# Split weights of two feed-forward layers kept in DRAM, in place of their sums alone

## The chip, the cores and the metric

The kernel runs on one core of one Trainium2 chip. The metric is the device time of one execution in microseconds; the median of several runs stands for a kernel. TensorE (PE) multiplies, VectorE (DVE), ScalarE (ACT) and GpSimd (POOL) work element by element, SyncE (SP) issues the DMA transfers between DRAM and SBUF, the memory on the chip.

## The reference

Attention with a memory term gives x, 2304 tokens by 512. Two feed-forward layers follow, all in float32:

```
g = x @ w_gate;  val = x @ w_val
x1 = (silu(g) * val) @ w_out          # 512 -> 1536 -> 512
h = x1 @ w_in                         # 512 -> 2048
g2 = h if h >= 1, 0 if h <= -1, else (h + 1)**2 / 4
out = g2 @ w_out2                     # 2048 -> 512
```

## The kernel before

The attention comes first, pair of heads by pair of heads. The feed-forward part is a hand-written schedule of 60 steps, in which each engine has its own program and waits for the others by semaphores.

**Tiling.** The tokens are cut into three superblocks of 768 for each layer: superblocks 0 to 2 are layer one (steps 0 to 35, 12 each), 3 to 5 are layer two (steps 36 to 59, 8 each). A step takes one block of weights of the up projection. It is multiplied by Strassen's scheme in Winograd's form: seven products of half size (`PRODUCTS`, L181) instead of eight. So the four quarters of a weight block need four sums besides (slots 4 to 7 of `wu_r`), and x needs four differences. The down projection works in groups of two tiles of weights (`wd_*`), 8 units of work a group, two groups behind the up projection (`LAG`).

**Three multiplications for one.** Float32 precision is reached by splitting each operand into a high part (rounded to fp32r) and a low part (the rest), and adding three matmuls: high by high, high by low, low by high (`three`, L1325). A matmul is 128x128 by 384 columns. A step has 42 matmuls for its products, and 24 (layer one, from step 4 on) or 48 (layer two) for units of the down projection. The last two groups follow after step 59.

**Splitting the weights.** The same weights serve three superblocks, and are loaded and split anew in each. For step u + 1, in step u: ScalarE writes the high parts of the up weights in three pieces (`up_high`, L718), GpSimd or VectorE subtract to get the low parts (`up_low`, L593 and L987; `pieces_of_pool`, L229, says which pieces are GpSimd's: one, but two or all three at a change of superblock). GpSimd and ScalarE do the same for the tiles of the down projection (`down_low` L604, `down_high` L727). `wu_l` and `wd_l` lie in the memory of `wu_r` and `wd_r`: the low part overwrites what was loaded.

**The sums.** `computed` (L204) tells in which steps GpSimd computes the four sums of the up weights (`up_sums_1`, `up_sums_2`): those of superblocks 0 and 3, and the first of superblocks 1 and 2. In the first of a layer SP stores them to DRAM (`keep_sums`, L470), and the splits that overwrite them wait for that store (L599, L992). In the others `load_up` (L461) loads the quarters and the kept sums.

**Buffers.** `wu_r`/`wu_l` has 3 buffers, `wu_h` 2, the tiles of the down projection 6 (3 groups). One SP program issues all loads and stores in the order of L510 to L523; a wait there holds up all that stands behind it.

**At a change of superblock** x of the next one is split too: seven high parts on ScalarE (`x_high`, L733), seven low parts on VectorE (`x_low`, L997), four differences on GpSimd (`x_sum`, L611, which waits at L618 for the last low part of the superblock before). VectorE also adds every unit of the down projection from PSUM into `xy` (`add_down`, L1111) and makes the low part of the hidden tiles (`hid_low`, L1095).

Of the kernel before, what the change touches and what calls it, by code (L numbers as in the profile page):

```python
# [1451 lines left out]
```

## Time and profile before

| | |
|---|---|
| median of 3 runs | 998.99 us (998.86 to 999.01) |
| profiled execution | 999.02 us |
| span of its trace | 997.2 us |
| TensorE, VectorE, ScalarE, GpSimd busy | 97%, 80%, 56%, 51% of the span |
| bytes moved by DMA | 116.13 MB, 116 GB/s over the span |
| granted TensorE clock | 1.000 of full speed |

The span runs from the first to the last instruction. Busy times of engines overlap. The records of matmuls overlap as well, since they are pipelined: the distance between the starts of two of them tells the pace, not their length.

### The profile page before, as it was taken

The numbers are of one execution on the slowest core, as the hardware profiler recorded it, in microseconds if no ns is written. First come the engines' busy times: TensorE is split into PE (matmuls) and PEld (weight loads), VectorE is DVE, ScalarE is ACT, GpSimd is POOL, SyncE is SP. The second block draws the span as 40 slices with busy tenths as digits, with TensorE's granted clock in tenths as the row PEclk, the third lists the DMA queues.
The fourth block names the chain that finished last, engine by engine and source line by source line (L and its number), as shares of the span: only waits on it lengthen the run. The fifth ranks groups of instructions, "written<-read, shape, count | busy, mean of one in ns | idle before, by whom it ended". The sixth has DMA issues, their size and how long they took to land.

```text
span 997.2 us, 19181 instructions
## 1 busy us (share of the span) xinstructions
PE 970.6 (97%) x6328; PEld 920.4 (92%) x6328; DVE 795.7 (80%) x1438; ACT 562.7 (56%) x1114; POOL 503.8 (51%) x407
## 2 busy tenths in 40 slices
PE   6999999999999999999999999999999999899998
PEld 4777777889999999999999999999989999899998
DVE  5888999567788677778667788888998888987776
ACT  5899998655446544454454454545654555545451
POOL 5677776176675233453234467576452526442331
PEclk9999999999999999999999999999999999999999
DMA  6545553333333332323333231323322431315211
GB/s 232 171 150 177 168 153 99 109 125 130 106 106 111 130 120 106 107 85 109 128 133 119 85 106 65 127 78 135 103 88 98 156 127 64 118 73 190 69 38 64
DMA packets 34782, 116.13 MB, mean 116 GB/s; under 512 B 4224, under 2 KB 4608, under 8 KB 34688
## 3 DMA queue, kind: packets, MB, share of 16 engines
q1 hardware_dynamic: 34544, 114.91, 34.2%
q8 instruction: 55, 0.90, 0.4%
q14 instruction: 39, 0.32, 0.1%
q10 hardware_dynamic: 144, 0.00, 0.0%
HBM read 100.14 MB, written 14.75 MB: 115 GB/s over the span
## 4 chain that ended last, share of the span: by engine, by line
PE 83%; DVE 6%; ACT 5%; issue 4%; DMA 1%; POOL 1%; SPq 0%; DVEq 0%; ACTq 0%; POOLq 0%
PE ps L1327 24%; PE ps L1329 23%; PE ps L1328 23%; PE ps L1302 5%; PE ps L1245 4%; ACT pt L716 3%; PE ps L1275 3%; DVE xt_l L1003 1%; DVE xy L1119 1%; DVE hid_l L1097 1%; DVE hid_r L1109 1%; ACT rown L695 1%; DMA qk<-qk_in 1%; DMA rbc<-rsums 0%; DVE negs L939 0%
## 5 line engine op out<-in xcount | busy, mean ns | idle before, releaser
L601 POOL TENSOR_TENSOR wu_l<-wu_r,wu_h 128x768 fp32r<-128x768 f32 (+1 forms) x75 | 142.0, 1901 | 396.3 <-ACT wu_h L725 396.3
L1327 PE MATMUL ps<-xt_h,wu_h 128*128 128x384 f32 x840 | 283.0, 337 | 5.9 <-DVE xt_l L1003 2.8
L1329 PE MATMUL ps<-xt_h,wu_l 128*128 128x384 f32 x840 | 280.8, 334 | 0.0
L1328 PE MATMUL ps<-xt_l,wu_h 128*128 128x384 f32 x840 | 280.7, 334 | 0.0
L1327 PE MATMUL ps<-hid_h,wd_h 128*128 128x384 f32 x672 | 226.2, 337 | 5.6 <-DVE xy L1119 5.3
L1329 PE MATMUL ps<-hid_h,wd_l 128*128 128x384 f32 x672 | 224.7, 334 | 0.0
L1328 PE MATMUL ps<-hid_l,wd_h 128*128 128x384 f32 x672 | 224.6, 334 | 0.0
L1119 DVE TENSOR_TENSOR xy<-xy,ps 128x384 f32<-128x384 f32 x288 | 157.2, 548 | 49.1 <-PE ps L1329 48.1
L803 ACT ACTIVATE hid_h<-hid_r 128x768 fp32r<-128x768 f32 x84 | 70.8, 843 | 199.1 <-DVE hid_r L1093 142.9
L1327 PEld LDWEIGHTS ps<-xt_h,wu_h 128*128 128x128 f32 x840 | 157.6, 188 | 13.7 <-issue 12.0
L1328 PEld LDWEIGHTS ps<-xt_l,wu_h 128*128 128x128 f32 x840 | 157.7, 188 | 0.0
L1329 PEld LDWEIGHTS ps<-xt_h,wu_l 128*128 128x128 f32 x840 | 157.7, 188 | 0.0
L607 POOL TENSOR_TENSOR wd_l<-wd_r,wd_h 128x512 fp32r<-128x512 f32 x84 | 136.6, 1639 | 15.1 <-ACT wd_h L730 13.9
L1327 PEld LDWEIGHTS ps<-hid_h,wd_h 128*128 128x128 f32 x672 | 126.1, 188 | 11.3 <-issue 6.9
L994 DVE TENSOR_TENSOR wu_l<-wu_r,wu_h 128x512 fp32r<-128x512 f32 x105 | 121.4, 1156 | 6.9 <-DMA kept<-wu_r 3.9
L1328 PEld LDWEIGHTS ps<-hid_l,wd_h 128*128 128x128 f32 x672 | 126.2, 188 | 0.0
L1329 PEld LDWEIGHTS ps<-hid_h,wd_l 128*128 128x128 f32 x672 | 126.1, 188 | 0.0
L725 ACT ACTIVATE wu_h<-wu_r 128x512 fp32r<-128x512 f32 (+1 forms) x180 | 118.9, 694 | 0.0
L1097 DVE TENSOR_TENSOR hid_l<-hid_r,hid_h 128x768 fp32r<-128x768 f32 x84 | 86.6, 1030 | 37.2 <-ACT hid_h L803 37.1
L695 ACT ACTIVATE rown<-negs,nmax 128x576 f32<-128x576 f32 (+3 forms) x128 | 77.1, 605 | 14.9 <-DVE nmax L939 14.9
L818 ACT ACTIVATE tmp<-hb,nhalf 128x768 f32<-128x768 f32 x48 | 45.1, 940 | 50.8 <-issue 45.9
L1103 DVE SCALAR_TENSOR_TENSOR tmp<-tmp 128x768 f32<-128x768 f32 x48 | 54.9, 1144 | 19.3 <-ACT tmp L818 18.7
(84 smaller groups left out, 1323.8 us busy)
## 6 DMA issues: line engine op xcount, KB each, us to landing
wu_r<-w_up SPq DMA_DIRECT2D x60, 512.0 KB, 4.6
wd_r<-w_down SPq DMA_DIRECT2D x42, 512.0 KB, 3.7
wu_r<-kept SPq DMA_DIRECT2D x38, 512.0 KB, 5.6
kept<-wu_r SPq DMA_DIRECT2D x19, 512.0 KB, 4.6
qk<-qk_in SPq DMA_DIRECT2D x15, 640.0 KB, 5.1
nat<-nat_in SPq DMA_DIRECT2D x16, 384.0 KB, 3.1
vm<-vm_in SPq DMA_DIRECT2D x16, 320.0 KB, 3.6
rbc<-rsums SPq DMA_DIRECT2D x32, 144.0 KB, 3.0
```

Of the source, the lines that this page charges most:

```text
L601: nc.gpsimd.tensor_tensor(wu_l[u % 3][:, a:b], wu_r[u % 3][:, a:b], wu_h[u % 2][:, a - 1:b - 1].bitcast(F32), ALU.subtract).then_inc(low_p ...
L607: nc.gpsimd.tensor_tensor(wd_l[:, t % 6], wd_r[:, t % 6], wd_h[:, t % 6].bitcast(F32), ALU.subtract).then_inc(wd_lo, 1)
L695: nc.scalar.activation(head_rows(j)[:, h + (i == 1), D:D + w], negs[:, t % NEGS, 0:w], ACT.Exp, bias=nmax[:, p % 2, k:k + 1], scale=-1.0, ...
L725: nc.scalar.activation(wu_h[u % 2][:, a - 1:b - 1], wu_r[u % 3][:, a:b], ACT.Copy).then_inc(wu_hi[n], 1)
L803: nc.scalar.activation(hid_h[:, t % 6], hid_r[:, t % 6], ACT.Copy).then_inc(hh_done, 1)
L994: nc.vector.tensor_tensor(wu_l[u % 3][:, a:b], wu_r[u % 3][:, a:b], wu_h[u % 2][:, a - 1:b - 1].bitcast(F32), ALU.subtract).then_inc(low_d ...
L1097: nc.vector.tensor_tensor(hid_l[:, t % 6], hid_r[:, t % 6], hid_h[:, t % 6].bitcast(F32), ALU.subtract).then_inc(hl_done, 1)
L1103: nc.vector.scalar_tensor_tensor(tmp[:, r], tmp[:, r], 1.0, tmp[:, r], ALU.min, ALU.mult).then_inc(s_done, 1)
L1119: nc.vector.tensor_tensor(y, y, o, ALU.add).then_inc(evac, 1)
L1327: nc.tensor.matmul(dst, w_hi, v_hi, start=start, stop=False, skip_group_check=onto)
L1328: nc.tensor.matmul(dst, w_hi, v_lo, start=False, stop=False, skip_group_check=onto)
L1329: return nc.tensor.matmul(dst, w_lo, v_hi, start=False, stop=stop, skip_group_check=onto)
```

## The change

In superblocks 0 and 3 the weights are loaded, summed and split as before. Then SP stores the high and low parts of all of them to four tensors in DRAM: seven slots for each up step (`keep_up`), two tiles for each group of the down projection (`keep_down`). In superblocks 1, 2, 4 and 5 the parts are read straight into the buffers from which TensorE takes them (`load_up_high`, the second branch of `load_up`, `load_down`), and no engine computes sums or splits for them; in these, TensorE waits for the loads at the first product of a step. The store of the sums (`keep_sums`) and its waits are gone. New waits: a load into a buffer waits until that buffer's store has landed; `up_high` and `down_high` wait until the store of the high part that they overwrite has landed. The first steps of superblocks 1 and 2 are no longer computed. The diff, cut to its core (the lines left out make the same conditions in the programs of ScalarE, VectorE and GpSimd, name semaphores and remove the old call of `keep_sums` in the attention):

```diff
@@ -104,7 +103,10 @@
 traw, o = place("traw", [P, 4, 2, HALF], F32, o)
-kept = nc.dram_tensor("kept", [S1 + S2, P, 4 * 2 * P], F32, kind="Internal").ap()
+kept_uh = nc.dram_tensor("kept_uh", [S1 + S2, P, 7 * 2 * P], F32, kind="Internal").ap()
+kept_ul = nc.dram_tensor("kept_ul", [S1 + S2, P, 7 * 2 * P], F32, kind="Internal").ap()
+kept_dh = nc.dram_tensor("kept_dh", [(NF1 + NF2) // 2, P, 2 * DM], F32, kind="Internal").ap()
+kept_dl = nc.dram_tensor("kept_dl", [(NF1 + NF2) // 2, P, 2 * DM], F32, kind="Internal").ap()
@@ -203,19 +209,15 @@
-    return superblock(u) in (0, NSB) or u < STEPS1 and u % S1 == 0
-def is_kept(u):
-    return superblock(u) in (0, NSB) and u > 0
+    return superblock(u) in (0, NSB)
+def computed_before(u):
+    return sum(computed(v) for v in range(u))
...
-    return 4 * sum(computed(v) for v in range(u))
-def kept_before(u):
-    return 16 * sum(is_kept(v) for v in range(u))
+    return 4 * computed_before(u)
@@ -223,7 +225,50 @@
-    return 16 * sum(1 if computed(v) else 2 for v in range(u % 3, u + 1, 3))
+    return 16 * (u // 3 + 1)
+def high_loads_until(u):
+    return 16 * sum(not computed(v) for v in range(u % 2, u + 1, 2))
+def kept_by(u):
+    return u % S1 if u < STEPS1 else STEPS1 + (u - STEPS1) % S2
+def stores_until(u, n):
+    return 16 * sum(computed(v) for v in range(u % n, u + 1, n))
+def down_computed(g):
+    return group_block(g) in (0, NSB)
+def down_computed_before(g):
+    return sum(down_computed(h) for h in range(g))
+def down_index(g):
+    return g % (NF1 // 2) if g < GROUPS1 else NF1 // 2 + (g - GROUPS1) % (NF2 // 2)
+def down_loads_until(g):
+    return 16 * sum(1 if down_computed(h) else 2 for h in range(g % 3, g + 1, 3))
+def down_kept_by(g):
+    return g % (NF1 // 2) if g < GROUPS1 else GROUPS1 + (g - GROUPS1) % (NF2 // 2)
+def down_stores_until(g):
+    return 16 * sum(down_computed(h) for h in range(g % 3, g + 1, 3))
+def tiles_split_until(t):
+    return 2 * down_computed_before(t // 2) + t % 2 + 1
@@ -458,28 +503,65 @@
     def load_up(u):
         at_least(sp, up, up_count(u - 3, 6))
+        if u >= 3 and computed(u - 3):
+            sp.wait_ge(up_kept_l[u % 3], stores_until(u - 3, 3))
         n = step_index(u)
-        sp.dma_start(wu_r[u % 3][:, 0:4], w_up[n].rearrange("p (k n) -> p k n", k=4)).then_inc(ld_up[u % 3], 16)
-        if not computed(u):
-            sp.wait_ge(sums_kept, kept_before(n + 1 if n < S1 else STEPS1 + n - S1 + 1))
-            sp.dma_start(wu_r[u % 3][:, 4:8], kept[n].rearrange("p (k n) -> p k n", k=4)).then_inc(ld_up[u % 3], 16)
-    def keep_sums(u):
-        sp.wait_ge(sums, sums_before(u) + 4)
-        sp.dma_start(kept[step_index(u)].rearrange("p (k n) -> p k n", k=4), wu_r[u % 3][:, 4:8]).then_inc(sums_kept, 16)
+        if computed(u):
+            sp.dma_start(wu_r[u % 3][:, 0:4], w_up[n].rearrange("p (k n) -> p k n", k=4)).then_inc(ld_up[u % 3], 16)
+        else:
+            sp.wait_ge(up_kept_l[kept_by(u) % 3], stores_until(kept_by(u), 3))
+            sp.dma_start(wu_l[u % 3][:, 1:8].bitcast(F32), kept_ul[n].rearrange("p (k n) -> p k n", k=7)).then_inc(ld_up[u % 3], 16)
+    def load_up_high(u):
+        at_least(sp, up, up_count(u - 2, 6))
+        if computed(u - 2):
+            sp.wait_ge(up_kept_h[u % 2], stores_until(u - 2, 2))
+        n = step_index(u)
+        sp.wait_ge(up_kept_h[kept_by(u) % 2], stores_until(kept_by(u), 2))
+        sp.dma_start(wu_h[u % 2][:].bitcast(F32), kept_uh[n].rearrange("p (k n) -> p k n", k=7)).then_inc(ld_uh[u % 2], 16)
+    def keep_up(u):
+        n = step_index(u)
+        for k in range(3):
+            sp.wait_ge(wu_hi[k], computed_before(u) + 1)
+        sp.dma_start(kept_uh[n].rearrange("p (k n) -> p k n", k=7), wu_h[u % 2][:].bitcast(F32)).then_inc(up_kept_h[u % 2], 16)
+        for k in range(3):
+            sp.wait_ge(*low_count(u, k))
+        sp.dma_start(kept_ul[n].rearrange("p (k n) -> p k n", k=7), wu_l[u % 3][:, 1:8].bitcast(F32)).then_inc(up_kept_l[u % 3], 16)
...
         at_least(sp, dn, UNITS * (g - 2))
-        n = g % (NF1 // 2) if g < GROUPS1 else NF1 // 2 + (g - GROUPS1) % (NF2 // 2)
-        s = 2 * (g % 3)
-        sp.dma_start(wd_r[:, s:s + 2], w_down[n].rearrange("p (k n) -> p k n", k=2)).then_inc(ld_dn[g % 3], 16)
+        if g >= 3 and down_computed(g - 3):
+            sp.wait_ge(dn_kept_l[g % 3], down_stores_until(g - 3))
+        n, s = down_index(g), 2 * (g % 3)
+        if down_computed(g):
+            sp.dma_start(wd_r[:, s:s + 2], w_down[n].rearrange("p (k n) -> p k n", k=2)).then_inc(ld_dn[g % 3], 16)
+            return
+        if down_computed(g - 3):
+            sp.wait_ge(dn_kept_h[g % 3], down_stores_until(g - 3))
+        by = down_kept_by(g)
+        sp.wait_ge(dn_kept_h[by % 3], down_stores_until(by))
+        sp.dma_start(wd_h[:, s:s + 2].bitcast(F32), kept_dh[n].rearrange("p (k n) -> p k n", k=2)).then_inc(ld_dn[g % 3], 16)
+        sp.wait_ge(dn_kept_l[by % 3], down_stores_until(by))
+        sp.dma_start(wd_l[:, s:s + 2].bitcast(F32), kept_dl[n].rearrange("p (k n) -> p k n", k=2)).then_inc(ld_dn[g % 3], 16)
+    def keep_down(g):
+        n, s = down_index(g), 2 * (g % 3)
+        sp.wait_ge(wd_hi, tiles_split_until(2 * g + 1))
+        sp.dma_start(kept_dh[n].rearrange("p (k n) -> p k n", k=2), wd_h[:, s:s + 2].bitcast(F32)).then_inc(dn_kept_h[g % 3], 16)
+        sp.wait_ge(wd_lo, tiles_split_until(2 * g + 1))
+        sp.dma_start(kept_dl[n].rearrange("p (k n) -> p k n", k=2), wd_l[:, s:s + 2].bitcast(F32)).then_inc(dn_kept_l[g % 3], 16)
@@ -512,10 +592,16 @@
             load_down(GROUPS1 + u - STEPS1)
-        if u > 0 and u + 1 < STEPS and is_kept(u + 1):
-            keep_sums(u + 1)
+        if u + 1 < STEPS and not computed(u + 1):
+            load_up_high(u + 1)
         if 0 < u and u + 2 < STEPS:
             load_up(u + 2)
+        if computed(u):
+            keep_up(u)
+        if u < STEPS1 and u % 2 == 1 and u >= 3 and down_computed((u - 3) // 2):
+            keep_down((u - 3) // 2)
+        if u >= STEPS1 + 2 and down_computed(GROUPS1 + u - STEPS1 - 2):
+            keep_down(GROUPS1 + u - STEPS1 - 2)
         if u > STEPS1 + S2 and (u - STEPS1) % S2 == LAG + 1:
@@ -593,17 +679,14 @@
         a, b = PIECES[n]
-        if computed(u):
-            pool.wait_ge(sums, sums_before(u) + (4, 3, 4)[n])
-        if n > 0 and is_kept(u):
-            pool.wait_ge(sums_kept, kept_before(u + 1))
-        pool.wait_ge(wu_hi[n], u + 1)
+        pool.wait_ge(sums, sums_before(u) + (4, 3, 4)[n])
+        pool.wait_ge(wu_hi[n], computed_before(u) + 1)
         nc.gpsimd.tensor_tensor(wu_l[u % 3][:, a:b], wu_r[u % 3][:, a:b], wu_h[u % 2][:, a - 1:b - 1].bitcast(F32),
...
-        pool.wait_ge(wd_hi, t + 1)
+        pool.wait_ge(wd_hi, tiles_split_until(t))
         nc.gpsimd.tensor_tensor(wd_l[:, t % 6], wd_r[:, t % 6], wd_h[:, t % 6].bitcast(F32),
@@ -719,14 +803,17 @@
         act.wait_ge(ld_up[u % 3], loads_until(u))
-        if computed(u):
-            at_least(act, sums, sums_before(u) + (0, 2, 4)[n])
+        at_least(act, sums, sums_before(u) + (0, 2, 4)[n])
         at_least(act, up, up_count(u - 2, 6))
+        if u >= 2 and computed(u - 2):
+            act.wait_ge(up_kept_h[u % 2], stores_until(u - 2, 2))
         nc.scalar.activation(wu_h[u % 2][:, a - 1:b - 1], wu_r[u % 3][:, a:b], ACT.Copy).then_inc(wu_hi[n], 1)
...
-        act.wait_ge(ld_dn[t // 2 % 3], 16 * (t // 6 + 1))
+        act.wait_ge(ld_dn[t // 2 % 3], down_loads_until(t // 2))
+        if t >= 6 and down_computed(t // 2 - 3):
+            act.wait_ge(dn_kept_h[t // 2 % 3], down_stores_until(t // 2 - 3))
         nc.scalar.activation(wd_h[:, t % 6], wd_r[:, t % 6], ACT.Copy).then_inc(wd_hi, 1)
@@ -879,7 +969,7 @@
             x_high(sb + 1, 0)
-        if more:
+        if split:
             if not fresh:
@@ -986,11 +1077,8 @@
         a, b = PIECES[n]
-        if computed(u):
-            dve.wait_ge(sums, sums_before(u) + 2 + n)
-        if is_kept(u):
-            dve.wait_ge(sums_kept, kept_before(u + 1))
-        dve.wait_ge(wu_hi[n], u + 1)
+        dve.wait_ge(sums, sums_before(u) + 2 + n)
+        dve.wait_ge(wu_hi[n], computed_before(u) + 1)
         nc.vector.tensor_tensor(wu_l[u % 3][:, a:b], wu_r[u % 3][:, a:b], wu_h[u % 2][:, a - 1:b - 1].bitcast(F32),
@@ -1334,8 +1423,12 @@
         sb = superblock(u)
-        pe.wait_ge(*low_count(u, piece_of(slot)))
-        pe.wait_ge(wu_hi[piece_of(slot)], u + 1)
+        if computed(u):
+            pe.wait_ge(*low_count(u, piece_of(slot)))
+            pe.wait_ge(wu_hi[piece_of(slot)], computed_before(u) + 1)
+        elif n == 0:
+            pe.wait_ge(ld_up[u % 3], loads_until(u))
+            pe.wait_ge(ld_uh[u % 2], high_loads_until(u))
         if u == first_of(sb):
@@ -1368,8 +1461,11 @@
         at_least(pe, hh_done, 2 * g + 2)
-        at_least(pe, wd_lo, 2 * g + 2)
-        at_least(pe, wd_hi, 2 * g + 2)
+        if down_computed(g):
+            pe.wait_ge(wd_lo, tiles_split_until(2 * g + 1))
+            pe.wait_ge(wd_hi, tiles_split_until(2 * g + 1))
+        else:
+            pe.wait_ge(ld_dn[g % 3], down_loads_until(g))
         at_least(pe, evac, n - 1)
...
```

## Rows read from the trace of the kernel before

**Rows 1.** Busy time of each engine, from the page.
```profile
PE 970.6 (97%) x6328; PEld 920.4 (92%) x6328; DVE 795.7 (80%) x1438; ACT 562.7 (56%) x1114; POOL 503.8 (51%) x407
```

**Rows 2.** Timeline of TensorE (start us, us long): first matmuls of steps, and the last.
```profile
184.86 0.44 PE L1327 MATMUL ps<-xt_h,wu_h 128*128 128x384 f32 x1
...
310.28 0.33 PE L1327 MATMUL ps<-xt_h,wu_h 128*128 128x384 f32 x1
...
322.52 0.33 PE L1327 MATMUL ps<-xt_h,wu_h 128*128 128x384 f32 x1
...
588.64 0.33 PE L1327 MATMUL ps<-xt_h,wu_h 128*128 128x384 f32 x1
...
718.54 0.33 PE L1327 MATMUL ps<-xt_h,wu_h 128*128 128x384 f32 x1
...
737.57 0.33 PE L1327 MATMUL ps<-xt_h,wu_h 128*128 128x384 f32 x1
...
867.50 0.33 PE L1327 MATMUL ps<-xt_h,wu_h 128*128 128x384 f32 x1
...
961.10 0.33 PE L1327 MATMUL ps<-xt_h,wu_h 128*128 128x384 f32 x1
...
976.85 0.41 PE L1327 MATMUL ps<-hid_h,wd_h 128*128 128x384 f32 x1
...
994.01 0.34 PE L1329 MATMUL ps<-hid_h,wd_l 128*128 128x384 f32 x1
```

**Rows 3.** Waits of TensorE (us in total, times, longest).
```profile
PE ps L1327 <- DVE xy L1119: 5.3, 10, 1.0
...
PE ps L1327 <- DVE xt_l L1003: 2.8, 5, 0.9
```

**Rows 4.** Timeline of VectorE in step 44.
```profile
721.12 0.95 DVE L1097 TENSOR_TENSOR hid_l<-hid_r,hid_h 128x768 fp32r<-128x768 f32 x1
...
722.86 0.54 DVE L1119 TENSOR_TENSOR xy<-xy,ps 128x384 f32<-128x384 f32 x1
...
723.32 2.14 DVE L1003 TENSOR_TENSOR xt_l<-traw,xt_h 128x768 fp32r<-128x768 f32 x1
...
725.39 2.03 DVE L1097 TENSOR_TENSOR hid_l<-hid_r,hid_h 128x768 fp32r<-128x768 f32 x1
```

**Rows 5.** Timeline of GpSimd in step 44.
```profile
722.34 6.22 POOL L601 TENSOR_TENSOR wu_l<-wu_r,wu_h 128x768 fp32r<-128x768 f32 x3 [4.62 <-ACT wu_h L725]
```

**Rows 6.** The costliest groups, from the page: splits of the weights.
```profile
L994 DVE TENSOR_TENSOR wu_l<-wu_r,wu_h 128x512 fp32r<-128x512 f32 x105 | 121.4, 1156 | 6.9 <-DMA kept<-wu_r 3.9
...
L601 POOL TENSOR_TENSOR wu_l<-wu_r,wu_h 128x768 fp32r<-128x768 f32 (+1 forms) x75 | 142.0, 1901 | 396.3 <-ACT wu_h L725 396.3
...
L607 POOL TENSOR_TENSOR wd_l<-wd_r,wd_h 128x512 fp32r<-128x512 f32 x84 | 136.6, 1639 | 15.1 <-ACT wd_h L730 13.9
...
L725 ACT ACTIVATE wu_h<-wu_r 128x512 fp32r<-128x512 f32 (+1 forms) x180 | 118.9, 694 | 0.0
```

**Rows 7.** Timeline of VectorE in step 2.
```profile
207.75 0.74 DVE L994 TENSOR_TENSOR wu_l<-wu_r,wu_h 128x512 fp32r<-128x512 f32 x1 [2.03 <-DMA kept<-wu_r]
```

**Rows 8.** Busy time by stretch; last columns: clock, DMA share, GB/s.
```profile
16.00:22.00 6.00, 4.92 (x38) 3.66 (x38) 5.13 (x17) 5.32 (x19) 5.08 (x7) 1.00 0.99 392
...
311.00:316.00 5.00, 4.91 (x28) 4.41 (x26) 4.80 (x7) 3.30 (x6) 0.00 (x0) 1.00 0.77 276
...
905.00:909.00 4.00, 4.00 (x25) 4.00 (x24) 3.16 (x5) 2.08 (x5) 3.80 (x3) 1.00 1.01 408
```

**Rows 9.** Timeline of SP in step 2.
```profile
204.77 0.33 SPq L473 DMA_DIRECT2D kept<-wu_r  x1
...
205.14 0.43 SPq L465 DMA_DIRECT2D wu_r<-w_up  x1
```

**Rows 10.** Timeline of GpSimd in step 47.
```profile
780.29 1.84 POOL L629 TENSOR_TENSOR traw<-xy 128x768 f32<-128x768 f32 x1
```

**Rows 11.** Timeline of VectorE in step 47.
```profile
780.95 2.00 DVE L1103 SCALAR_TENSOR_TENSOR tmp<-tmp 128x768 f32<-128x768 f32 x1
```

More of the change, by code:

```diff
@@ L235, in low_count @@
         def low_count(u, n):
-            pool = [n in pieces_of_pool(v - 1) for v in range(u + 1)]
-            return (low_pool if pool[u] else low_dve)[n], sum(p == pool[u] for p in pool)
+            pool = {v: n in pieces_of_pool(v - 1) for v in range(u + 1) if computed(v)}
+            return (low_pool if pool[u] else low_dve)[n], sum(x == pool[u] for x in pool.values())
         def raw_sum(sb, n):
@@ L665, in _ @@
                 for n in pieces_of_pool(u):
-                    if 0 < u and u + 1 < STEPS:
+                    if 0 < u and u + 1 < STEPS and computed(u + 1):
                         up_low(u + 1, n)
                 for t in down_tiles(u):
-                    down_low(t)
+                    if down_computed(t // 2):
+                        down_low(t)
                 if 0 < u and u + 2 < STEPS and computed(u + 2):
@@ L839, in _ @@
                     x_high(sb + 1, 0)
-                if u > 0:
+                if u > 0 and computed(u + 1):
                     up_high(u + 1, 1)
@@ L845, in _ @@
                 for t in down_tiles(u):
-                    down_high(t)
-                if u > 0:
+                    if down_computed(t // 2):
+                        down_high(t)
+                if u > 0 and computed(u + 1):
                     up_high(u + 1, 2)
@@ L862, in _ @@
                 more = u + 1 < STEPS
+                split = more and computed(u + 1)
                 ends = more and superblock(u + 1) != sb
@@ L881, in _ @@
                     x_high(sb + 1, 0)
-                if more:
+                if split:
                     if not fresh:
@@ L891, in _ @@
                 for t in down_tiles(u):
-                    down_high(t)
+                    if down_computed(t // 2):
+                        down_high(t)
                 if ends:
@@ L1142, in _ @@
                     x_low(sb, 5)
-                if u > 0 and 1 not in pieces_of_pool(u):
+                if u > 0 and computed(u + 1) and 1 not in pieces_of_pool(u):
                     up_low(u + 1, 1)
@@ L1147, in _ @@
                     add_down(n)
-                if u > 0 and 2 not in pieces_of_pool(u):
+                if u > 0 and computed(u + 1) and 2 not in pieces_of_pool(u):
                     up_low(u + 1, 2)
@@ L1166, in _ @@
                 more = u + 1 < STEPS
+                split = more and computed(u + 1)
                 ends = more and superblock(u + 1) != sb
@@ L1181, in _ @@
                     x_low(sb, 4)
-                if more and 1 not in pieces_of_pool(u):
+                if split and 1 not in pieces_of_pool(u):
                     up_low(u + 1, 1)
@@ L1192, in _ @@
                 add_down(units[3])
-                if more and 2 not in pieces_of_pool(u):
+                if split and 2 not in pieces_of_pool(u):
                     up_low(u + 1, 2)
```

12 lines of the change are left out of this document (7 added, 5 removed).

## The prediction

> **What bounds the kernel now.** First the busy shares: TensorE is at 97%, the next engine at 80% [rows 1]. A busy share is no proof for pipelined matmuls, so next the timeline of TensorE. Its 4536 feed-forward matmuls run from 184.86 to 994.01 us [rows 2]. Steps 53 to 58 show the pace when nothing is late: 961.10 - 867.50 = 93.60 us for 6 x 90 matmuls, 0.1733 us each [rows 2]. At that pace 4535 intervals are 786.1 us; the stretch is 809.15 us. So TensorE is held up for 23.1 us, and no change beside the matmuls can bring more. Nothing is said of the attention before, which the change leaves as it is, one early transfer apart.
>
> Where the 23.1 us lie, by superblock (length less matmuls x 0.1733, all starts from [rows 2]): superblock 0, where the weights of layer one are split for the first time, 125.42 - 696 x 0.1733 = 4.8. Superblocks 1 and 2 together, 278.36 - 1584 x 0.1733 = 3.8; of it step 12 alone 12.24 - 11.44 = 0.8. Superblock 3, 129.90 - 124.80 = 5.1. Superblocks 4 and 5, 258.31 - 249.60 = 8.7; of it step 44 alone 19.03 - 15.60 = 3.4, and step 52 repeats it. The tail, 17.16 - 16.47 = 0.7. The waits of TensorE in feed-forward name VectorE: 5.3 us for the adds into xy and 2.8 us for the low parts of x [rows 3]. So VectorE is what comes late.
>
> Why is it late in step 44, where it has no weight to split (there GpSimd takes all three pieces)? VectorE's subtract of 128x768 took 0.95 us at 721.12. The same at 725.39 took 2.03, and the low part of x at 723.32 took 2.14, while GpSimd ran three subtracts without a break from 722.34 on [rows 4, 5]. The adds that read PSUM stay at 0.54 beside it [rows 4]. So GpSimd's work on the weights stretches VectorE's operations on SBUF alone.
>
> **What goes away.** In the four superblocks that are no longer computed go two thirds of the splits. Group by group [rows 6]: VectorE keeps 37 of 105 `up_low`, 68 x 1.16 = 79 us gone; GpSimd keeps 23 of 75 and 28 of 84 `down_low`, 52 x 1.90 + 56 x 1.64 = 191 us gone; ScalarE keeps 60 of 180 `up_high`, 120 x 0.69 = 83 us gone, and 56 `down_high`. None of this is on TensorE, so only what it does to the 23.1 us counts.
>
> Superblocks 1 and 2: apart from the two change steps, 3.8 - 1.6 = 2.2 us go, less 0.2 in step 35, which still splits for step 36. Of the 0.8 in a change step most is the chain from the last product to the low part of x, which stays; I take 0.25 each as gained. Sum 2.5 of 3.8.
>
> Superblocks 4 and 5: without GpSimd, the two operations of step 44 lose 1.19 and 1.08 us, and the three low parts of x behind them their share; that is the size of the step's 3.4. The steps 47 to 50 lose two `up_low` each. I keep 1.1 us as left and count 7.6 of 8.7.
>
> Superblock 0: in steps 2 and 3 VectorE waited for the store of the sums before it could overwrite them (2.03 us in step 2 [rows 7]). That wait falls: the new stores follow the split. Bound 0 to 2 us for each of two steps; TensorE felt it through one add, and I take 0.65 each, 1.3. Superblock 3 and the tail keep theirs.
>
> **What is added, all of it on the SP queue.** A step's seven slots are 917,504 bytes a part. In superblock 0 each step stores 1.84 MB and loads 0.52, and every second step loads 0.52 and stores 1.05 for a group: 6.3 MB in two steps of 11.44 us. Later steps load 1.84 MB, and 1.05 every second step. What can the queue move? With a backlog the rows show 392 GB/s for loads (16 to 22 us) and 408 for the output's store (905 to 909); without one, 276 (311 to 316) [rows 8]. The new queue has a backlog, so I take 400 and keep 276 for the range. At 400 two steps need 15.7 of 22.9 us. TensorE kept its pace under 408 GB/s (25 matmuls in 4 us [rows 8]), so more traffic slows no matmul: nothing, with that cover.
>
> The new waits. `load_up(u + 2)` now waits until the low part of step u - 1 has landed in DRAM; behind it on SP stand `keep_up(u)`, `keep_down` and the next `load_down`. A store's fixed part: issued at 204.77, it let VectorE go at 207.75 [rows 7, 9], 2.98 us, less 0.52 MB at 408 = 1.3, leaves 1.7 us. From the first issue at about 188.6 us: (0.52 + 1.84) MB at 400 is 5.9, plus 1.7, so the load for step 3 goes out near 196.3, and 7.6 us later, at 203.9, the one for step 4, which before went out at 205.14 [rows 9]. So at 400 nothing is late; at 276 it would be 10.2 us a turn, the load for step 4 at 209, four us late, and GpSimd's sums, ScalarE's and VectorE's splits wait behind it. I take 0; range 0 to 7 us. ScalarE's `up_high` waits for the high store of two steps earlier, which is queued ahead of that low store and lands first.
>
> In the other superblocks TensorE waits at product 0 for both loads. The worst is an even step: 1.05 MB and the high part, 1.97 MB, issued at its start, are there after 5.0 + 1.7 us, at 276 after 8.8, of 11.44. Layer two has 15.6. Nothing.
>
> Sum: 2.5 + 7.6 + 1.3 = 11.4 us. The profiled execution took 999.02 us, 0.03 above the median of the runs, so the forecast is 999.02 - 11.4 = 987.6 for both. Differences of 0.2%, 2 us, are about what a measurement of this kernel tells from none.
>
> **Rivals.** *Slower: the SP queue becomes the bound in superblock 0.* Until the high part for step 13 is there it must move 12 x 1.84 + 5 x 1.05 (stores) + 15 x 0.52 + 1.05 + 4 x 0.92 (loads) = 39.8 MB, from 188.3 to about 320.8 (322.52 before [rows 2] less 1.7), in 132.5 us. Six times, at even steps, nothing is queued behind the waiting load: 6 x 1.7 = 10 us. At 400 that is 110 us, 22 to spare; at 276, 154, so TensorE waits 22 us in steps 1 to 13, and 999 + 22 - 11 = 1010. It decides below 39.8 / (132.5 + 11.4 - 10) = 297 GB/s. For it: 276 is a real row. Against: that window had a DMA share of 0.77, the queue was not full, and stores show 408 [rows 8]. Chance 0.09. *No difference:* rates near 300 give back what is gained, 997 to 1001; 0.05.
>
> *The four differences of x bunch up.* GpSimd's `x_sum` no longer stand behind splits; all four for the next superblock can run as soon as the last low part of x is done, late in step 44. One of 1.84 us at 780.29 stretched VectorE's operation at 780.95 to 2.00 [rows 10, 11]. Four of them are 7.4 us in a step where VectorE has least to spare, worth up to half of that, in both layers: 991. By the Trainium skill, page "SBUF — State Buffer", section "SBUF: two separate sides", the two engines share a port pair as an exclusive lock, held for a whole instruction, against VectorE operations with two SBUF inputs; the rows agree (2.03 against 0.95, PSUM adds at 0.54 [rows 4]), and by the page the bunch would stop each such operation in turn. Chance 0.08.
>
> *VectorE's own work is the limit* at steps 44 and 52, and the stretching only filled idle time. Then 2 x 3.4 us of the 7.6 stay, and the time is 994. Against it: the operations in [rows 4] follow each other without a gap. Chance 0.08.
>
> **Numbers.** The forecast has 0.70: 987.6, and from 985.4 (all of superblocks 4 and 5 and 2 us more in superblock 0 gained) to 990. With the two smaller gains the range is 985.4 to 994.5 and holds 0.86. Faster 0.86, same 0.05, slower 0.09.
>
> **What would show it.** Right: steps 44 and 52 within 0.8 us of 15.60, no stretched subtracts there, superblock 3 still some 5 us over, DMA shares near 1 in superblock 0 with SP's waits ending before TensorE's. Wrong: a wait of TensorE for a DMA at the start of steps 12 to 14, or steps 1 to 4 longer than now because the sums start late; a queue under 300 GB/s with a backlog; or step 44 unchanged with GpSimd idle.

## The result and the profile after

The changed kernel takes 990.39 us in the median of 4 runs (990.22 to 991.28), the kernel before on the same chip 998.92 (998.60 to 999.01). The ratio is 0.9917 with an interval from 0.9900 to 0.9934: faster by 8.5 us, where 11.4 were forecast. The profiled execution took 990.56 us, 988.7 of them in the span, at a granted clock of 1.000.

The page of the changed kernel, busy time of the engines and bytes moved (beside [rows 1]):

```profile
PE 965.2 (98%) x6328; PEld 921.2 (93%) x6328; DVE 709.6 (72%) x1370; ACT 463.1 (47%) x938; POOL 309.8 (31%) x291
...
DMA packets 46156, 204.72 MB, mean 207 GB/s; under 512 B 5488, under 2 KB 5872, under 8 KB 46064
```

The costliest groups of the changed kernel, splits of the weights (beside [rows 6]):

```profile
L684 POOL TENSOR_TENSOR wu_l<-wu_r,wu_h 128x768 fp32r<-128x768 f32 (+1 forms) x23 | 44.1, 1922 | 79.8 <-ACT wu_h L810 79.7
L690 POOL TENSOR_TENSOR wd_l<-wd_r,wd_h 128x512 fp32r<-128x512 f32 x28 | 43.6, 1568 | 42.6 <-ACT wd_h L817 42.3
...
L810 ACT ACTIVATE wu_h<-wu_r 128x512 fp32r<-128x512 f32 (+1 forms) x60 | 39.7, 692 | 0.6 <-PE ps L1418 0.6
L1082 DVE TENSOR_TENSOR wu_l<-wu_r,wu_h 128x512 fp32r<-128x512 f32 x37 | 37.3, 1009 | 1.4 <-ACT wu_h L810 1.4
```

The counts are those worked out from the code: 23, 28, 60 and 37. GpSimd lost 194 us of busy time, ScalarE 100, VectorE 86; the time fell by 8.5. Busy time off the critical path is not worth its length. What counts stands in the timeline of TensorE in the changed kernel (beside [rows 2]):

```profile
184.47 0.44 PE L1416 MATMUL ps<-xt_h,wu_h 128*128 128x384 f32 x1
...
309.80 0.33 PE L1416 MATMUL ps<-xt_h,wu_h 128*128 128x384 f32 x1
...
321.60 0.33 PE L1416 MATMUL ps<-xt_h,wu_h 128*128 128x384 f32 x1
...
585.07 0.33 PE L1416 MATMUL ps<-xt_h,wu_h 128*128 128x384 f32 x1
...
715.35 0.33 PE L1416 MATMUL ps<-xt_h,wu_h 128*128 128x384 f32 x1
...
731.97 0.33 PE L1416 MATMUL ps<-xt_h,wu_h 128*128 128x384 f32 x1
...
749.73 0.33 PE L1416 MATMUL ps<-xt_h,wu_h 128*128 128x384 f32 x1
...
843.33 0.33 PE L1416 MATMUL ps<-xt_h,wu_h 128*128 128x384 f32 x1
...
858.93 0.33 PE L1416 MATMUL ps<-xt_h,wu_h 128*128 128x384 f32 x1
...
968.13 0.33 PE L1416 MATMUL ps<-hid_h,wd_h 128*128 128x384 f32 x1
...
985.47 0.34 PE L1418 MATMUL ps<-hid_h,wd_l 128*128 128x384 f32 x1
```

Read as in the prediction, each stretch less its matmuls x 0.1733 us:

| stretch | lost before | lost after | gain | forecast |
|---|---|---|---|---|
| superblock 0 (184.47 to 309.80) | 4.8 | 4.7 | 0.1 | 1.3 |
| superblocks 1, 2 (to 585.07) | 3.8 | 0.7 | 3.1 | 2.5 |
| superblock 3 (to 715.35) | 5.1 | 5.5 | -0.4 | 0 |
| superblocks 4, 5 (to 968.13) | 8.7 | 3.2 | 5.5 | 7.6 |
| tail (to 985.47) | 0.7 | 0.9 | -0.2 | 0 |

So 8.2 us of the 23.1 came back and 14.9 stayed. Two terms were missed: superblock 0 gave 0.1 in place of 1.3, and superblocks 4 and 5 gave 2.1 less. Of the 3.2 that they still lose, step 44 has 731.97 - 715.35 - 15.60 = 1.0, and step 45, which lost nothing before, 749.73 - 731.97 - 15.60 = 2.2. Steps 47 to 50 and step 52 (843.33 to 858.93) are at 15.60.

**Step 45.** VectorE in steps 44 and 45 of the changed kernel (beside [rows 4]):

```profile
719.54 0.95 DVE L1091 TENSOR_TENSOR xt_l<-traw,xt_h 128x768 fp32r<-128x768 f32 x1
720.41 0.95 DVE L1185 TENSOR_TENSOR hid_l<-hid_r,hid_h 128x768 fp32r<-128x768 f32 x1
...
727.99 2.25 DVE L1191 SCALAR_TENSOR_TENSOR tmp<-tmp 128x768 f32<-128x768 f32 x1
730.16 0.54 DVE L1207 TENSOR_TENSOR xy<-xy,ps 128x384 f32<-128x384 f32 x1
730.63 2.12 DVE L1197 TENSOR_TENSOR hid_r<-hb,tmp 128x768 f32<-128x768 f32 x1
...
733.13 2.13 DVE L1191 SCALAR_TENSOR_TENSOR tmp<-tmp 128x768 f32<-128x768 f32 x1
...
735.65 2.12 DVE L1185 TENSOR_TENSOR hid_l<-hid_r,hid_h 128x768 fp32r<-128x768 f32 x1
```

and GpSimd in the same stretch (beside [rows 5]):

```profile
723.92 3.70 POOL L690 TENSOR_TENSOR wd_l<-wd_r,wd_h 128x512 fp32r<-128x512 f32 x2 [12.06 <-ACT wd_h L817]
727.58 1.84 POOL L712 TENSOR_TENSOR traw<-xy 128x768 f32<-128x768 f32 x1
729.57 2.37 POOL L712 TENSOR_TENSOR traw<-xy,traw 128x768 f32<-128x768 f32 x1
731.89 2.56 POOL L712 TENSOR_TENSOR traw<-xy 128x768 f32<-128x768 f32 x1
734.41 2.55 POOL L712 TENSOR_TENSOR traw<-xy,traw 128x768 f32<-128x768 f32 x1
```

The two operations that took 2.14 and 2.03 us now take 0.95, as forecast. Then the four `x_sum` run without a break from 727.58 to 736.96, after the last low part of x and right behind GpSimd's last two splits of down weights, and four VectorE operations take 2.12 to 2.25. They seem to take turns. The one begun at 730.63 lies in a difference that ends at 731.94; 0.95 more gives 732.89, and it ended at 732.75. The next difference begins at 731.89; 1.84 from 732.75 gives 734.59, and it ended at 734.45. The add that reads PSUM stays at 0.54. That is what the lock in the Trainium skill, page "SBUF — State Buffer", section "SBUF: two separate sides", would give.

**Superblock 0.** SP, the loads of the quarters for steps 3, 4 and 5 in the changed kernel, and one of down weights between them (beside [rows 9]):

```profile
196.72 0.33 SPq L514 DMA_DIRECT2D wu_r<-w_up  x1
...
198.05 1.50 SPq L548 DMA_DIRECT2D wd_r<-w_down  x1
...
206.67 0.33 SPq L514 DMA_DIRECT2D wu_r<-w_up  x1
...
215.32 0.33 SPq L514 DMA_DIRECT2D wu_r<-w_up  x1
```

GpSimd there, the first sum for step 4:

```profile
211.03 0.74 POOL L668 TENSOR_TENSOR wu_r<-wu_r 128x256 f32<-128x256 f32 x1 [1.71 <-DMA wu_r<-w_up]
```

Busy time by stretch (beside [rows 8]; the last columns are clock, DMA share and GB/s):

```profile
200.00:212.00 12.00, 11.53 (x65) 10.91 (x64) 7.55 (x11) 6.45 (x12) 8.57 (x9) 1.00 0.83 319
212.00:224.00 12.00, 10.38 (x59) 9.78 (x58) 9.45 (x12) 7.56 (x13) 10.04 (x10) 1.00 0.85 312
190.00:310.00 120.00, 117.08 (x668) 115.24 (x667) 87.48 (x122) 61.27 (x102) 73.90 (x61) 1.00 0.83 305
```

and the first waits of TensorE in step 3, from its timeline:

```profile
215.12 0.41 PE L1416 MATMUL ps<-xt_h,wu_h 128*128 128x384 f32 x1 [0.91 <-ACT u2s L875]
...
217.10 0.44 PE L1416 MATMUL ps<-xt_h,wu_h 128*128 128x384 f32 x1 [0.70 <-POOL wu_l L684]
```

The load for step 4 went out at 206.67, not at 203.9. GpSimd waited 1.71 us for it, its sums came late, ScalarE's high parts behind them, and TensorE lost 0.91 and 0.70 us in step 3, where the kernel before lost 0.19 and 0.24 at the same two places. In return the two waits of TensorE for `hb`, a block that VectorE adds up from the products, 0.43 us each in steps 3 and 4 before, are gone.

Waits of TensorE over the whole execution (beside [rows 3]):

```profile
PE ps L1416 <- DVE xy L1207: 4.9, 11, 1.1
...
PE ps L1416 <- DVE xt_l L1091: 0.4, 1, 0.4
```

The wait for the low parts of x fell from 2.8 to 0.4 us; that for `xy` is still there, but it is another one: what is left of it lies outside the steps 47 to 50 and 52, which are at pace now.

### The profile page after: what moved, and what is told of

It is laid out like the page before. It is cut to its first block, busy times and chain, and to the rows that moved or that the text cites. A ratio compares the mean times of both kernels' runs of the same rounds, so it can differ in the third digit from the quotient of the medians.

```text
span 988.7 us, 18774 instructions
## 1 busy us (share of the span) xinstructions
PE 965.2 (98%) x6328; PEld 921.2 (93%) x6328; DVE 709.6 (72%) x1370; ACT 463.1 (47%) x938; POOL 309.8 (31%) x291
## 2 busy tenths in 40 slices
DMA packets 46156, 204.72 MB, mean 207 GB/s; under 512 B 5488, under 2 KB 5872, under 8 KB 46064
## 4 chain that ended last, share of the span: by engine, by line
PE 84%; ACT 5%; issue 4%; DVE 4%; DMA 2%; POOL 1%; ACTq 0%; DVEq 0%; SPq 0%; POOLq 0%
PE ps L1416 24%; PE ps L1417 24%; PE ps L1418 24%; PE ps L1391 5%; PE ps L1334 4%; ACT pt L800 3%; PE ps L1364 3%; DMA kept_ul<-wu_l 1%; DVE xt_l L1091 1%; DVE xy L1207 1%; ACT rown L779 1%; DMA betas<-beta 1%; DVE hid_l L1185 1%; ACT tmp L905 0%; DMA wu_r<-w_up 0%
## 5 line engine op out<-in xcount | busy, mean ns | idle before, releaser
L875 ACT ACTIVATE u2s<-ps 128x384 f32<-128x384 f32 x60 | 29.4, 491 | 96.8 <-PE ps L1418 96.8
L1191 DVE SCALAR_TENSOR_TENSOR tmp<-tmp 128x768 f32<-128x768 f32 x48 | 54.3, 1131 | 23.4 <-ACT tmp L905 23.1
L684 POOL TENSOR_TENSOR wu_l<-wu_r,wu_h 128x768 fp32r<-128x768 f32 (+1 forms) x23 | 44.1, 1922 | 79.8 <-ACT wu_h L810 79.7
L1030 DVE CUSTOM_DVE_ANT_0 negs<-ps,mask 128x576 f32<-128x576 f32 (+3 forms) x128 | 63.6, 552 | 4.7 <-PE ps L1334 4.6
L1162 DVE TENSOR_TENSOR hb<-u2s,ps 128x384 f32<-128x384 f32 x60 | 33.1, 552 | 46.4 <-PE ps L1418 44.4
```

What stands on the lines that cost most here:

```text
L684: nc.gpsimd.tensor_tensor(wu_l[u % 3][:, a:b], wu_r[u % 3][:, a:b], wu_h[u % 2][:, a - 1:b - 1].bitcast(F32), ALU.subtract).then_inc(low_p ...
L1030: nc.vector.tensor_tensor_reduce(negs[:, t % NEGS, 0:w], psf[:, col:col + w], mask[:, S - w:S], -(float(D) ** -0.5), 3.0e38, ALU.add, ALU. ...
L1191: nc.vector.scalar_tensor_tensor(tmp[:, r], tmp[:, r], 1.0, tmp[:, r], ALU.min, ALU.mult).then_inc(s_done, 1)
```

## The experiments

Times are medians; the ratio is to the kernel before in the same batch, with its interval. "Lost" is the stretch of TensorE from its first to its last feed-forward matmul less 786.1 us, from one profile: 23.1 before, 14.9 with the change. All kernels are the changed one with the edit shown; e4 to e8 and e12 have the edit of e1 besides. Added stand-ins work on tiles that nobody reads.

| kernel | median | ratio [interval] | lost |
|---|---|---|---|
| the change | 990.39 | 0.9917 [0.9900, 0.9934] | 14.9 |
| e1_gate_xsum | 986.79 | 0.9874 [0.9859, 0.9889] | 11.1 |
| e2_early_store | 989.13 | 0.9898 [0.9883, 0.9913] | 13.7 |
| e3_gate_and_early | 985.74 | 0.9864 [0.9847, 0.9880] | 9.9 |
| e4_gpsimd_busy | 990.33 | 0.9907 [0.9893, 0.9922] | 14.2 |
| e5_vector_busy | 986.69 | 0.9873 [0.9859, 0.9888] | 10.9 |
| e6_vector_gpsimd_busy | 996.30 | 0.9966 [0.9955, 0.9977] | 23.9 |
| e7_gpsimd_earlier | 994.56 | 0.9954 [0.9939, 0.9969] | 18.7 |
| e8_scalar_gpsimd_busy | 992.06 | 0.9927 [0.9911, 0.9944] | 15.8 |
| e9_up_only | 987.12 | 0.9875 [0.9860, 0.9890] | 11.7 |
| e10_high_twice | 1008.94 | 1.0099 [1.0082, 1.0116] | 31.7 |
| e11_up_only_early | 986.58 | 0.9866 [0.9851, 0.9881] | 9.8 |
| e12_three_busy | 992.22 | 0.9920 [0.9903, 0.9937] | 18.5 |

In three of these profiles "lost" holds time at TensorE's lower clock. Busy time by stretch of e6 (the third column from the end is the clock):

```profile
217.73:221.14 3.41, 3.41 (x12) 3.41 (x12) 1.68 (x3) 0.49 (x1) 2.07 (x2) 0.50 0.88 336
320.13:323.54 3.41, 3.41 (x13) 3.41 (x12) 3.34 (x5) 0.84 (x1) 0.04 (x1) 0.50 0.35 145
460.08:463.49 3.41, 3.41 (x12) 3.41 (x12) 2.52 (x5) 0.79 (x1) 0.56 (x1) 0.50 0.34 141
```

A clock of 0.50 is the lower of two levels, 1.2 and 2.4 GHz. From 218.06 to 220.62 TensorE started a matmul every 0.32 us there, not every 0.1733, so a stretch of 3.41 us costs some 1.6 us (an estimate from these two rates). Before each of the three it had waited, 1.22 and 0.54 us before the first, 1.76 and 1.79 before the others. e12 has one such stretch (217.54 to 220.95), e10 two (211.04 to 214.46 and 333.92 to 340.75). The other kernels of the table have none in the feed-forward part.

### Do the four differences cost what steps 44 and 45 lose?

e1_gate_xsum lets each `x_sum` wait for a product of its own step, so that one runs per step:

```diff
                     if u + ahead < STEPS and superblock(u + ahead) != superblock(u + ahead - 1):
+                        pool.wait_ge(up, up_count(u, 4))
                         x_sum(superblock(u + ahead), n)
```

> The four differences of x are held back until product 4 of the step in which they stand in GpSimd's program, so that they run one a step. Theory (the bunch of four in steps 44 and 45 holds up VectorE): the 3.1 us that TensorE loses in these two steps go, 990.4 - 3.1 = 987.3 us, and steps 47 to 50 lose at most 0.3 us each. Rival (VectorE's own work is the limit at a change of superblock): the stalls stay somewhere in steps 44 to 46, 990.4 us.

TensorE in its timeline, first matmuls of steps 44, 45 and 46:

```profile
714.77 0.33 PE L1417 MATMUL ps<-xt_h,wu_h 128*128 128x384 f32 x1
...
730.37 0.33 PE L1417 MATMUL ps<-xt_h,wu_h 128*128 128x384 f32 x1
...
745.97 0.33 PE L1417 MATMUL ps<-xt_h,wu_h 128*128 128x384 f32 x1
```

and GpSimd, where the first two differences now lie:

```profile
771.17 1.85 POOL L712 TENSOR_TENSOR traw<-xy 128x768 f32<-128x768 f32 x1 [44.12 <-PE ps L1419]
786.77 1.85 POOL L712 TENSOR_TENSOR traw<-xy,traw 128x768 f32<-128x768 f32 x1 [13.75 <-PE ps L1419]
```

Both steps are at 15.60. The gain is 3.6 us by the medians, of which 1.0 + 2.2 lie in these two steps, and 0.5 in step 42. The bunch is shown to be the cause of what steps 44 and 45 lose. In layer one the same four ran without a break from 319.18 us on and steps there lost nothing more, so the term is one of layer two alone.

### Is superblock 0 held by the queue's first turns?

e2_early_store moves the stores of steps 0 and 1, whose parts are ready in the attention, ahead into its pairs 11 to 14:

```diff
...
+            EARLY_KEEP = {11: (0, 0), 12: (0, 1), 13: (1, 0), 14: (1, 1)}
...
                 read_r(p - 1)
+                if p in EARLY_KEEP:
+                    keep_part(*EARLY_KEEP[p])
...
-                if computed(u):
+                if computed(u) and u > 1:
                     keep_up(u)
```

> The parts of steps 0 and 1 are stored during the attention (pairs 11 to 14), where the queue is idle half of the time, not in steps 0 and 1. Theory (in steps 1 to 3 the loads of the next weights wait behind these stores, and step 3 loses 1.2 us by it): the load for step 3 goes out near 194 us and not 196.7, that for step 4 before 204 and not 206.7, superblock 0 loses 3.4 us instead of 4.7, 989.1 us. Rival (the first steps are bound by the chain from product to split alone): 990.4 us. If the attention feels the stores, its end moves from 184.5 us by up to 1 us.

SP in its timeline, loads for steps 3 and 4:

```profile
195.15 0.33 SPq L514 DMA_DIRECT2D wu_r<-w_up  x1
...
203.80 0.33 SPq L514 DMA_DIRECT2D wu_r<-w_up  x1
```

The load for step 4 goes out 2.9 us earlier, and step 3 loses 1.0 us instead of 2.1. The gain in the median is 1.3 us; the two intervals overlap, so the size rests on the profile. The loss follows the load: in e4 below, which lacks this edit, the load for step 4 happened to go out at 205.38, and step 3 lost 1.1 us there. The feed-forward part begins 1.0 us later in this profile (185.49), which has a clock of 0.50 from 16.59 to 20.01 in the attention; with the same early stores it begins at 184.54 in e3 and 184.34 in e11, so the attention is not seen to pay for them. e3_gate_and_early has both edits.

> Both edits. If the two losses are separate: 990.4 - 3.1 - 1.3 = 986.0 us. If one hides the other: no better than the better of the two alone, about 987.3 us.

On the same chip it is 1.05 us below e1 and 3.4 below e2: the two add up. It is the fastest of all, 1.4% below the kernel before.

### Was it GpSimd, or VectorE's own work?

Five kernels on top of e1 put work back without the data. e4_gpsimd_busy gives GpSimd its subtracts, after product 2 of each step:

```diff
...
+                if again:
+                    pool.wait_ge(up, up_count(u, 2))
...
+                    if again:
+                        spare(256 * (PIECES[n][1] - PIECES[n][0]))
...
+                    else:
+                        spare(512)
```

> As with the differences held back, and GpSimd again runs subtracts of the old sizes in superblocks 1, 2, 4 and 5, on a tile of its own that nobody reads or waits for; VectorE and ScalarE have no splits there. Theory (GpSimd's operations stretch VectorE's, and that was most of the 12.5 us of stalls in these superblocks before): steps 44 and 52 lose some 3 us each again, 987.3 + 6 = 993 us (991 to 995). Rival (what counted was the work taken from VectorE and ScalarE): 987.3 us, nothing changes.

e5_vector_busy gives VectorE a 128x512 subtract wherever a split of its own stood:

```diff
...
+                if again(u) and n not in pieces_of_pool(u):
+                    nc.vector.tensor_tensor(spare_v[:], spare_v[:], spare_v[:], ALU.subtract).then_inc(done_v, 1)
```

> As with the differences held back, and VectorE again runs subtracts of 128x512 on a tile of its own where its splits were in superblocks 1, 2, 4 and 5 (two a step, none at a change of superblock layer two); GpSimd and ScalarE have none. Theory (VectorE has room for its own splits as long as GpSimd is quiet): at most 0.4 us more than the 986.8 us without them. Rival (it was VectorE's own work that made it late in steps 19 to 21, 31 to 33 and 47 to 50): these steps lose 0.28 us each again, 989.6 us or more.

What single steps lose against the pace, read from the timeline of TensorE in each kernel:

| step | before | change | e1 | e4 | e5 | e6 | e7 | e8 |
|---|---|---|---|---|---|---|---|---|
| 12 | 0.8 | 0.4 | 0.3 | 1.4 | 0.3 | 3.7 | 2.2 | 0.7 |
| 19, 20, 21 (each) | 0.3 | 0 | 0 | 0 | 0 | 0 | 0 | 0 |
| 24 | 0.8 | 0.4 | 0.4 | 1.4 | 0.4 | 3.7 | 2.1 | 0.7 |
| 44 | 3.4 | 1.0 | 0 | 1.2 | 0 | 2.0 | 2.0 | 2.2 |
| 45 | 0 | 2.2 | 0 | 0 | 0 | 0 | 0 | 0 |
| 47 to 50 (each) | 0.3 | 0 | 0 | 0 | 0 | 0 | 0 | 0 |
| 52 | 3.7 | 0 | 0 | 0.7 | 0 | 1.6 | 1.6 | 1.8 |

VectorE's splits alone cost nothing: 986.69 against 986.79, no step longer. (At steps 44 and 52 VectorE had no splits before either, so e5 says nothing of these two.) GpSimd's in e4 costs 3.5 us, less than the theory had in steps 44 and 52; the stand-ins came later in the step than the real subtracts. So e7_gpsimd_earlier has them after product 1 (`up_count(u, 1)`), e6_vector_gpsimd_busy adds VectorE's to that, and e8_scalar_gpsimd_busy has them released by copies on ScalarE in the place and order of the old `up_high`.

> VectorE's and GpSimd's subtracts both back, on tiles of their own (GpSimd's start after product 1 of a step). Theory (late is VectorE where its two splits are stretched by GpSimd's): the 2.9 us of steps 19 to 21, 31 to 33 and 47 to 50 return, beside what GpSimd alone costs at the changes of superblock (3.5 us in the run before): 993 us (991.5 to 995). If it is no more than GpSimd alone, 990.3 us, the stalls in these steps had another cause.

> GpSimd's subtracts alone, two units of work earlier in the step (after product 1 and not 2), near the time that they had in step 44 before. Theory (what GpSimd costs depends on which of VectorE's operations it meets; before, it met the low part of x for product 3 and the hidden tile's): step 44 loses more than the 1.2 us of the later start, 2 us or more, 991.5 us (990.5 to 993). If GpSimd's share is what the later start showed: 990.3 us, 1.2 us in step 44 and 0.6 in step 52.

> ScalarE's copies (128x512) and GpSimd's subtracts back in the old order, GpSimd's waiting for ScalarE's as the splits did, both on tiles of their own; VectorE has none. At the changes of layer two this is the work of before, but for the weights themselves. Theory (these two make the stalls of steps 44 and 52): both lose 3 us or more again, with 1 us in steps 12 and 24: 986.8 + 7 = 994 us (992.5 to 995.5). Rival (the loads from DRAM in place of splits, the weights' own waits, took the stalls away): 990.3 us or less.

In e7 the subtracts start at the time of [rows 5]; GpSimd, then VectorE of e7 in step 44:

```profile
722.24 5.21 POOL L759 TENSOR_TENSOR spare_p<-spare_p 128x768 f32<-128x768 f32 x3 [6.86 <-PE ps L1441]
```

```profile
723.08 1.76 DVE L1114 TENSOR_TENSOR xt_l<-traw,xt_h 128x768 fp32r<-128x768 f32 x1
724.76 1.79 DVE L1208 TENSOR_TENSOR hid_l<-hid_r,hid_h 128x768 fp32r<-128x768 f32 x1
```

VectorE is stretched to 1.76 and 1.79 us where [rows 4] have 2.14 and 2.03. Of the 7.1 us that steps 44 and 52 lost before, e7 brings back 3.6 and e8, with ScalarE's copies as well, 4.0: GpSimd's subtracts alone make half of the two stalls. The moment matters as much as the work, since e4 brings back 1.9 with the same subtracts. The stand-ins took 5.21 us for three, the real ones 6.22. They read one tile twice and are shorter by themselves: the shortest of 128x768 takes 1.47 us, the shortest real one 1.84. VectorE takes its turn behind either. The first stand-in ends at 724.02 in e7; 0.95 more gives 724.97, and the low part of x ended at 724.84. Before, the first real subtract ends at 724.65; 0.95 more gives 725.60, and it ended at 725.46. So the stand-ins are too light for the whole stall; that the rest of the 7.1 us is the difference in their length is likely and not shown. e8, with the subtracts in their old order, also gives steps 12 and 24 their old loss. e7 does not: its subtracts cost 3.6 us in these two steps, where the kernel before lost 1.6 in all.

e6 seems to lose 1.5 us more than e7 in each of steps 12 and 24 and in superblock 0. These are its three stretches at a clock of 0.50. TensorE's waits in steps 12 and 24 are those of e7 (1.76 and 1.79 us in both), and the one of e6's ten executions with a granted clock of 1.000 took 994.09 us, where e7's four took 994.10 to 995.98. So VectorE's splits cost nothing beside GpSimd's stand-ins either. The expectations of e4, e6, e7 and e8 gave ranges, and all four medians lie outside them; e6's would lie inside at a clock of 1.000.

What stays at zero everywhere are the steps 19 to 21 and 47 to 50. e12_three_busy therefore adds VectorE's subtracts to e8, in layer one:

```diff
...
+                    nc.vector.tensor_tensor(tmp[:, 0, 0:512], tmp[:, 0, 0:512], tmp[:, 0, 0:512], ALU.subtract).then_inc(done_v, 1)
```

> As the run with ScalarE and GpSimd busy (992.1 us), with VectorE's subtracts of 128x512 back too, in layer one only (in a tile that layer one doesn't use). Theory (in steps 19 to 21 and 31 to 33 VectorE was late because its two splits met GpSimd's splits and differences of x): these six steps lose 0.28 us each again, 1.7 us in all, 993.8 us. Rival (they had another cause, which no busy engine brings back): 992.1 us and no stall in these steps.

Steps 19 to 21 lose nothing here either. In step 19, VectorE and GpSimd of the kernel before, which started the step at 391.16, then VectorE of e12, which started it at 392.81:

```profile
399.11 2.04 DVE L994 TENSOR_TENSOR wu_l<-wu_r,wu_h 128x512 fp32r<-128x512 f32 x1
```

```profile
398.77 1.84 POOL L629 TENSOR_TENSOR traw<-xy 128x768 f32<-128x768 f32 x1
```

```profile
400.76 1.35 DVE L1278 TENSOR_TENSOR tmp<-tmp 128x512 f32<-128x512 f32 x1
```

Before, the split lay in the difference that GpSimd ended at 400.61, and it ended 10.00 us into the step. VectorE's last add of the step followed without a gap and began 10.85 us into it, 0.25 later than in the changed kernel (10.60), and TensorE lost 0.3. In e12 GpSimd's stand-ins ahead of the difference are shorter, the stand-in of VectorE ends 9.30 us into the step, and VectorE is idle for 0.37 us before that add. So the trace of before says that these steps were late by a split behind a difference, but the stand-ins are too light to test it, and no experiment here shows it. In step 47 the moment of the difference changed: [rows 10, 11] have it beside a VectorE operation that takes 2.00 us, and in e1 it is done at 773.02, before that operation, which starts at 773.75 and takes 0.95. That this freed steps 47 to 50 is read from the traces too, not tried.

### Is it the down weights too?

e9_up_only keeps the up weights alone; those of the down projection are loaded and split anew in each superblock, as before the change:

```diff
         def down_computed(g):
-            return group_block(g) in (0, NSB)
+            return True
...
-                if u < STEPS1 and u % 2 == 1 and u >= 3 and down_computed((u - 3) // 2):
-                    keep_down((u - 3) // 2)
```

> One part of the change alone: the up weights are kept split, the tiles of the down projection are loaded and split anew in every superblock as before (56 subtracts of 128x512 on GpSimd and 56 copies on ScalarE more than the changed kernel, half the bytes for the down weights). The differences of x stand behind these subtracts again and don't bunch up. Theory (GpSimd's operations cost at the changes of superblock, the rest is hidden): the bunch's 3.1 us are saved, 1 to 2 us are lost by the subtracts, 988.5 us (987 to 990.5). Rival (half of the gain belongs to the down weights, as half of the removed subtracts do): 993 us or more.

Half of the change is faster than all of it: 987.12. Steps 44, 45 and 52 are at 15.60 with no gate: the splits of the down weights stand between the differences again and hold them apart. It also moves 175.36 MB in place of 204.72. e11_up_only_early adds the early stores.

> The up weights alone are kept, and the parts of steps 0 and 1 are stored during the attention. Theory (the two gains are separate, as the two before were): 987.1 - 1.2 = 985.9 us, level with the 985.7 us of the changed kernel with both edits, at a quarter less traffic. If the down weights kept were worth something by themselves, it stays above that version by more than 1 us.

At 986.58 and a loss of 9.8 us it is level with e3. So keeping the down weights brings nothing that can be measured here.

### How near was the slower rival?

e10_high_twice stores every high part a second time, to a tensor that nobody reads, 0.92 MB a step more in superblocks 0 and 3:

```diff
...
+                sp.dma_start(twice[n].rearrange("p (k n) -> p k n", k=7), wu_h[u % 2][:].bitcast(F32)).then_inc(up_kept_h[u % 2], 16)
```

> Every high part of the up weights is stored twice, the second time to a tensor that nobody reads: 0.92 MB more a step in superblocks 0 and 3, nothing else changed. In the changed kernel the queue moved 305 GB/s at a busy share of 0.83 between 190 and 310 us, 367 at full share; with the double store it would need 305 + 80 = 385. Theory (superblock 0 was near the queue's limit): steps 2 to 4 start late and TensorE waits for weights at the change to superblock 1, 8 us or more in all, 998 us or more. Rival (the queue has room to 400 GB/s and more): 992.5 us or less, from the later loads of the first steps alone.

Busy time by stretch of e10, then the start of step 13 in its TensorE:

```profile
190.00:310.00 120.00, 109.93 (x612) 106.51 (x611) 75.70 (x113) 56.26 (x94) 72.12 (x60) 0.99 0.90 344
```

```profile
337.41 0.66 PE L1418 MATMUL ps<-xt_h,wu_h 128*128 128x384 f32 x1 [5.77 <-issue]
```

Slower than before by 9.5 us: superblock 0 loses 14.5 us in place of 4.7, and TensorE waits 5.8 us at the start of step 13. The load of the high part for step 13 landed at 337.32, just before that matmul. Some 3 us of the loss is the clock, 0.50 from 211.04 to 214.46 and from 333.92 to 340.75 (an estimate by the two rates above). So the rival's mechanism is real, at the place that the prediction gave it, and 0.92 MB a step more than the change has brings it on.

## Why the prediction was right or wrong

- **Direction and place: right.** Forecast 987.6, measured 990.4, inside the range of 985.4 to 994.5, but 0.4 above the narrower one of the forecast itself (to 990). Steps 44 and 52 were freed of GpSimd's splits of the up weights (step 52 at 15.60, the two stretched VectorE operations at 0.95 us), superblocks 1 and 2 gave 3.1 us for 2.5 (0.4 in each change step where 0.25 was taken), superblock 3 stayed some 5 us over. Three of its own signs failed: step 44 was 1.0 us over 15.60 and not within 0.8, step 3 was 0.5 longer than before, and the DMA share in superblock 0 was 0.83 and not near 1.
- **VectorE's own work as the limit: refuted.** Step 52 of the changed kernel and step 44 of e1 run at 15.60, and VectorE does the same there as before, since it had no weight to split in these steps. Elsewhere e5 puts its subtracts back at no cost. GpSimd's cost 3.5 us in e4 and 7.9 in e7, and 5.4 with ScalarE's copies in e8 (against e5 in the same batch, e4 against e1); in steps 44 and 52 alone it is 1.9, 3.6 and 4.0.
- **"The four differences of x bunch up": a term, not an alternative.** The prediction named the mechanism, gave it 0.08 and left it out of the sum. It happened, at 3.2 to 3.6 us where "up to half" of 7.4 was said, but in layer two alone. Its cause could be read in the program: with the splits gone, nothing stood ahead of the differences but the last low part of x. With 3.6 in the sum, the forecast would have been 991.2. The 1.1 us that the sum kept as left in superblocks 4 and 5 went the other way: e1 loses nothing there. So the two errors hid each other in part, and that the total came as near as 2.8 us is luck to that extent.
- **The queue in superblock 0: mis-sized.** "At 400 nothing is late" failed. The load for step 3 went out at 196.72 (forecast 196.3; the first transfer ahead of it was issued at 187.71 and not at 188.6, which hid a part of the lower rate), the one for step 4 9.95 us later instead of 7.6. The turn of the sum held 0.52 + 1.84 MB and left out the load of down weights issued at 198.05, 0.52 MB more. With it 2.88 MB in 9.95 - 1.7 us is 349 GB/s; the next turn, without it, is 2.36 MB in 8.65 - 1.7 us, 340. Both speak for some 345 GB/s in place of 400. (That this load shares the turn with the store ahead of it is read from these two rates, not tried.) The delay cost about what the fallen wait of VectorE gave, 1.2 us, and e2 gives it back.
- **The slower rival: rightly placed, and not far.** 305 GB/s moved over superblock 0, and it was to decide below 297. But the queue was 0.83 busy, not near 1, so 305 is not its limit: e10 moved 344.

## What to carry to other kernels

Price work taken from an engine off the critical path by the operations that it stretches on the engine for which the critical one waits, not by its busy time, and then ask what the emptied engine will do early: work that was held apart only by its predecessors bunches up at its first allowed moment, and one wait can put the spacing back. Try the parts of a change alone, since one of them may bring all of the gain at less traffic. Sum a queue's turn transfer by transfer, those of other buffers too, at a rate below that of a stream in one direction.
